# First transform of a long convolution: even and odd parts as two matmuls into the PSUM halves, evicted whole by ScalarE; VectorE multiplies and folds

## The reference, cut to what matters

```python
# B, S, D = 2, 11456, 128
h_filt = (np.maximum(pos_emb @ w1, 0.0) @ w2) * np.exp(-0.01 * pos)[:, None]
u = x * v
Uf = np.fft.rfft(u, n=2 * S, axis=1)
Hf = np.fft.rfft(h_filt, n=2 * S, axis=0)
y = np.fft.irfft(Uf * Hf[None, :, :], n=2 * S, axis=1)[:, :S, :]
attn_out = x * y
# then: expert layer 1 on attn_out, expert layer 2 on its result
```

## Time and profile before

| what | us |
|---|---|
| median of 3 runs | 2397.1 |
| the profiled execution | 2405.55 |
| its span (first to last instruction) | 2403.3 |
| filter stage | until about 80 |
| `spectra`, first half | 79.8 to 187.3 |
| `products`, first half | 187.3 to about 331 |
| `spectra`, second half | 331.0 to 431.2 |
| DVE busy over the span | 1359.6 (57%) |
| PE busy over the span | 1995.1 (83%) |

### The profile page before, as it was taken

One profiled execution on the slowest core, in us unless ns is written; L12 is line 12 of the kernel. 1 busy time (PEld: TensorE's weight loads), 2 busy tenths in 40 slices (PEclk: granted clock), 3 DMA queues, 4 the chain that ended last, 5 costly groups with the idle time before them and its releaser, 6 DMA issues. The chain is left out here.

```text
span 2403.3 us, 35753 instructions
## 1 busy us (share of the span) xinstructions
PE 1995.1 (83%) x9744; PEld 1639.1 (68%) x9744; DVE 1359.6 (57%) x3564; ACT 998.3 (42%) x2175; POOL 775.4 (32%) x738
## 2 busy tenths in 40 slices
PE   6577878686657675199999999999679999999996
PEld 4474567454647564178888887888558888888885
DVE  2397859774435353256666665666535555555552
ACT  3363333232222121045455554545335555555553
POOL 2143215330344555403232322222403333333333
PEclk9689998897667766599999999999889999999998
DMA  6657866786645563355555555555256666666662
GB/s 203 179 150 255 270 181 170 221 279 204 206 156 197 184 227 120 139 191 192 205 190 205 189 203 188 188 207 179 92 191 225 223 221 224 219 220 224 223 219 79
DMA packets 164823, 471.11 MB, mean 196 GB/s; under 512 B 24634, under 2 KB 80750, under 8 KB 135113
## 3 DMA queue, kind: packets, MB, share of 16 engines
q1 hardware_dynamic: 129416, 385.43, 49.0%
q0 software_dynamic: 24064, 61.17, 7.5%
q10 hardware_dynamic: 11264, 23.57, 3.2%
HBM read 365.29 MB, written 109.49 MB: 198 GB/s over the span
## 5 line engine op out<-in xcount | busy, mean ns | idle before, releaser
L1151 DVE SCALAR_TENSOR_TENSOR m_hid<-m_pH,m_hid 128x512 fp32r<-128x512 f32 x832 | 574.5, 691 | 406.5 <-ACT m_hid L1105 330.3
L1105 ACT ACTIVATE m_hid<-m_pH 128x512 fp32r<-128x512 f32 x832 | 501.0, 603 | 614.4 <-PE m_pH L1033 585.4
L1223 POOL DMA_INDIRECT rows<-m_rows,m_idx x208 | 204.0, 981 | 522.9 <-DVEq L1190 464.0
L1031 PE MATMUL m_pH<-m_xT,m_w 128*128 128x512 f32 x832 | 353.2, 425 | 11.4 <-DVE m_hid L1151 5.1
L1227 POOL DMA_INDIRECT out_dram<-m_rows,m_token x208 | 203.9, 980 | 434.2 <-ACT m_rows L1119 384.5
L1033 PE MATMUL m_pH<-m_xT,m_w 128*128 128x512 f32 x832 | 327.1, 393 | 0.0
L1032 PE MATMUL m_pH<-m_xT,m_w 128*128 128x512 f32 x832 | 326.9, 393 | 0.0
L1044 PE MATMUL m_pO<-m_hid,m_w 128*128 128x512 f32 x832 | 326.4, 392 | 0.0
L1046 PE MATMUL m_pO<-m_hid,m_w 128*128 128x512 f32 x832 | 326.0, 392 | 0.0
L1045 PE MATMUL m_pO<-m_hid,m_w 128*128 128x512 f32 x832 | 324.1, 390 | 0.0
L927 POOL DMA_INDIRECT rows<-oi_rows,oi_idx x192 | 194.3, 1012 | 226.7 <-ACT oi_raw_logits L880 129.2
(11 more groups left out here) (154 smaller groups left out, 2669.7 us busy)
## 6 DMA issues: line engine op xcount, KB each, us to landing
m_w<-halves_w SPq DMA_DIRECT2D x104, 1024.0 KB, 5.0
m_w<-halves_next_w SPq DMA_DIRECT2D x104, 1024.0 KB, 5.1
m_x<-rows SPq DMA_DIRECT2D x104, 264.0 KB, 4.3
pr_mats<-in_inner_dram SPq DMA_DIRECT2D x92, 256.0 KB, 3.9
inner_back<-pr_c SPq DMA_DIRECT2D x92, 256.0 KB, 3.5
oi_C<-inner_back SPq DMA_DIRECT2D x32, 728.0 KB
halves_w<-pr_parts POOLq DMA_DIRECT2D x16, 1024.0 KB
halves_next_w<-oi_parts ACTq DMA_DIRECT2D x32, 512.0 KB
```

The source lines that it names most:

```text
L1031: nc.tensor.matmul(out, high, xT[:, s % 2, 0], start=True, stop=False)
L1105: nc.scalar.activation(hid[:, s % 2, c, 0], pH[:, c % 2], ACT.Relu).then_inc(H_high, 1)
L1151: nc.vector.scalar_tensor_tensor(hid[:, s % 2, c, 1], pH[:, c % 2], 0.0, hid[:, s % 2, c, 0].bitcast(F32), ALU.max, ALU.subtract).then_inc ...
L1223: pool.indirect_dma_start(next_rows, bass.IndirectOffsetOnAxis(r.idx[:, s, t:t + 1], 0), rows[:, s, t, :], None, bounds_check=E * CAP + TI ...
```

## The change

The even and odd parts of a channel become two matmuls of 64 output partitions each, into partitions 0 to 63 and 64 to 127 of the same PSUM columns. The odd one has its own constant (`W[:, 1]`, the sine columns with their sign first, then minus the cosines), so that real and imaginary parts lie in the same columns for both, and the sign needs no instruction. ACT then evicts each part over all 128 partitions, in the form of the second half for both halves. DVE no longer evicts: it multiplies x by v, one signal chunk ahead of its folds, and folds. POOL has nothing to do in this stage. Filter and signal chunks alternate, one filter chunk and then two of signals, and `us` has 4 buffers. `W` is twice as long.

```diff
--- before.py
+++ after.py
@@ -186,81 +186,77 @@
 
 def spectra(nc, half, x, v, h_d, outer_d, A):
 
-    R = 3
+    R, UR = 4, 3
     with ExitStack() as ctx:
         sb, ps, sem = makers(nc, ctx, f"sp{half}")
-        xs, vs, us = (sb(n, [JP, R, CD, 2, HS]) for n in ("x", "v", "u"))
-        W = sb("W", [JP, 2 * K1])
+        xs, vs = (sb(n, [JP, UR, CD, 2, HS]) for n in ("x", "v"))
+        us = sb("u", [JP, R, CD, 2, HS])
+        W = sb("W", [JP, 2, 2 * K1])
         pA = ps("pA", [ST, 2, 4, 512])
         W_in = sem("W_in")
-        h_in, x_in = ([sem(f"{n}{s}") for s in range(R)] for n in ("h_in", "x_in"))
-        multiplied, folded = sem("multiplied"), sem("folded")
-        A_ready, even_out, odd_out = sem("A_ready"), sem("even_out"), sem("odd_out")
+        h_in, x_in = [sem(f"h_in{s}") for s in range(R)], [sem(f"x_in{s}") for s in range(UR)]
+        multiplied, folded, A_ready, A_out = sem("multiplied"), sem("folded"), sem("A_ready"), sem("A_out")
+
+        def is_filter(c):
+            return c % 3 == 0
+
+        def signal(c):
+
+            return c - c // 3 - 1
+
+        def place(u):
+
+            return u + u // 2 + 1
 
         def columns(c, part):
 
-            if c < CHUNKS_H:
-                at = WU + part * HD + c * CD
+            if is_filter(c):
+                at = WU + part * HD + c // 3 * CD
             else:
-                b, m = divmod(c - CHUNKS_H, CHUNKS_H)
+                b, m = divmod(signal(c), CHUNKS_H)
                 at = part * B * HD + b * HD + m * CD
             return slice(at, at + CD)
 
-        def move(c, rows, src, part):
-
-            outs = A[rows, :, columns(c, part)]
-            ins = pA[rows, c % 2, :, 0:4 * K1].rearrange("p a (t w) -> p a t w", t=2)[:, :, :, src * K1:(src + 1) * K1]
-            if half == 0:
-                return outs.rearrange("p k (a t) -> p a t k", t=2), ins
-            return outs.rearrange("p k (a t) -> p k a t", t=2), ins.rearrange("p a t w -> p w a t")
-
         block = ctx.enter_context(nc.Block())
 
         @block.sync
         def _(sp):
-            sp.dma_start(W[:, :], outer_d).then_inc(W_in, 16)
+            sp.dma_start(W[:, :, :].rearrange("p e w -> p (e w)"), outer_d).then_inc(W_in, 16)
+
             def load_filter(c):
                 if c >= R:
                     sp.wait_ge(A_ready, c - R + 1)
                 sp.dma_start(us[:, c % R].rearrange("p d e s -> p (d e s)"),
-                             h_d[half, :, c * CD * ST:(c + 1) * CD * ST]).then_inc(h_in[c % R], 16)
+                             h_d[half, :, c // 3 * CD * ST:(c // 3 + 1) * CD * ST]).then_inc(h_in[c % R], 16)
 
             def load_signals(u):
                 b, m = divmod(u, CHUNKS_H)
-                if u >= R:
-                    sp.wait_ge(folded, 2 * (u - R + 1))
+                if u >= UR:
+                    sp.wait_ge(folded, 2 * (u - UR + 1))
                 for dst, src in ((xs, x), (vs, v)):
-                    sp.dma_start(dst[:, u % R].rearrange("p d e s -> p (d e s)"),
-                                 src[b, half, :, m * CD * ST:(m + 1) * CD * ST]).then_inc(x_in[u % R], 16)
-
-            for c in range(CHUNKS_H):
-                load_filter(c)
-                if c < R:
-                    load_signals(c)
-            for u in range(R, CHUNKS_U):
-                load_signals(u)
-
-        @block.gpsimd
-        def _(pool):
-            for u in range(CHUNKS_U):
-                pool.wait_ge(x_in[u % R], 32 * (u // R + 1))
-                nc.gpsimd.tensor_tensor(xs[:, u % R], xs[:, u % R], vs[:, u % R], ALU.mult).then_inc(multiplied, 1)
+                    sp.dma_start(dst[:, u % UR].rearrange("p d e s -> p (d e s)"),
+                                 src[b, half, :, m * CD * ST:(m + 1) * CD * ST]).then_inc(x_in[u % UR], 16)
+
+            for c in range(CHUNKS_1):
+                if is_filter(c):
+                    load_filter(c)
+                else:
+                    load_signals(signal(c))
 
         @block.tensor
         def _(pe):
             pe.wait_ge(W_in, 16)
             for c in range(CHUNKS_1):
-                if c < CHUNKS_H:
-                    pe.wait_ge(h_in[c % R], 16 * (c // R + 1))
+                if is_filter(c):
+                    pe.wait_ge(h_in[c % R], 16 * len([k for k in range(0, c + 1, 3) if k % R == c % R]))
                 else:
-                    pe.wait_ge(folded, 2 * (c - CHUNKS_H + 1))
+                    pe.wait_ge(folded, 2 * (signal(c) + 1))
                 if c >= 2:
-                    pe.wait_ge(even_out, 2 * (c - 1))
-                    pe.wait_ge(odd_out, 2 * (c - 1))
+                    pe.wait_ge(A_out, 2 * (c - 1))
                 for d in range(CD):
-                    last = nc.tensor.matmul(pA[:, c % 2, d // 2, d % 2 * 2 * K1:(d % 2 + 1) * 2 * K1],
-                                            us[:, c % R, d].rearrange("p e s -> p (e s)"), W[:, :],
-                                            start=True, stop=True)
+                    for e in range(2):
+                        last = nc.tensor.matmul(pA[e * HS:(e + 1) * HS, c % 2, d // 2, d % 2 * 2 * K1:(d % 2 + 1) * 2 * K1],
+                                                us[:, c % R, d, e], W[:, e], start=True, stop=True)
                 last.then_inc(A_ready, 1)
 
         @block.scalar
@@ -268,27 +264,31 @@
             for c in range(CHUNKS_1):
                 act.wait_ge(A_ready, c + 1)
                 for part in range(2):
-                    dst, src = move(c, slice(0, HS), part, part)
-                    nc.scalar.activation(dst, src, ACT.Copy).then_inc(even_out, 1)
+                    src = pA[:, c % 2, :, 0:4 * K1].rearrange("p a (t w) -> p a t w", t=2)
+                    nc.scalar.activation(A[:, :, columns(c, part)].rearrange("p k (a t) -> p k a t", t=2),
+                                         src[:, :, :, part * K1:(part + 1) * K1].rearrange("p a t w -> p w a t"),
+                                         ACT.Copy).then_inc(A_out, 1)
 
         @block.vector
         def _(dve):
-            def fold(c):
-                u = c - CHUNKS_H
+            def multiply(u):
+                dve.wait_ge(x_in[u % UR], 32 * (u // UR + 1))
+                nc.vector.tensor_tensor(xs[:, u % UR], xs[:, u % UR], vs[:, u % UR], ALU.mult).then_inc(multiplied, 1)
+
+            def fold(u):
+                c = place(u)
                 dve.wait_ge(multiplied, u + 1)
-                dve.wait_ge(A_ready, c - R + 1)
+                if c >= R:
+                    dve.wait_ge(A_ready, c - R + 1)
                 for e, op in enumerate((ALU.add, ALU.subtract)):
-                    nc.vector.tensor_tensor(us[:, c % R, :, e], xs[:, u % R, :, 0], xs[:, u % R, :, 1],
+                    nc.vector.tensor_tensor(us[:, c % R, :, e], xs[:, u % UR, :, 0], xs[:, u % UR, :, 1],
                                             op).then_inc(folded, 1)
 
-            for c in range(CHUNKS_1):
-                if CHUNKS_H <= c + 2 < CHUNKS_1:
-                    fold(c + 2)
-                dve.wait_ge(A_ready, c + 1)
-                dst, src = move(c, slice(HS, ST), 1, 0)
-                nc.vector.tensor_copy(dst, src).then_inc(odd_out, 1)
-                dst, src = move(c, slice(HS, ST), 0, 1)
-                nc.vector.tensor_scalar(dst, src, -1.0, None, ALU.mult).then_inc(odd_out, 1)
+            multiply(0)
+            for u in range(CHUNKS_U):
+                if u + 1 < CHUNKS_U:
+                    multiply(u + 1)
+                fold(u)
 
 
 def products(nc, half, A, mats_d, c_d, weights, halves_d):
@@ -1314,7 +1314,7 @@
     number = np.where(at < S, at, NOWHERE) + np.where(at < S, S, 0) * np.arange(B)[:, None, None, None]
     return {
         "inner": f(np.stack([there, there.transpose(0, 2, 1)], axis=2).reshape(K1, ST, 2 * ST)),
-        "outer": f(np.concatenate([np.cos(outer) * real, -np.sin(outer) * real], axis=1)),
+        "outer": f(np.concatenate([np.cos(outer), -np.sin(outer), -np.sin(outer), -np.cos(outer)], axis=1) * real),
         "outer_inv": f(np.stack([weight * np.cos(back), -weight * np.sin(back), weight * np.sin(back)], axis=1) * real[:, 0]),
         "window": f(np.repeat(window, FO, axis=0).reshape(2 * FO, GROUPS, 2, GC)),
         "consts": f(np.concatenate([np.eye(128), np.ones((128, 128)), np.triu(np.ones((128, 128)), 1)], axis=1)),
```

## The result

The changed kernel takes 2442.05 us (median of 4 runs, 2430.51 to 2447.61) against 2400.09 for the kernel before (2391.37 to 2405.64): a ratio of 1.0196 with a 95% interval from 1.0142 to 1.0251. It is 42 us slower. The forecast was 2419, slower, with a range from 2390 to 2475: the direction was right, the loss about twice the 22 us that were forecast.

The account below looks back on a forecast made before the run. It took DVE to bound the first half, and folds slowed beside POOL's multiply in the second; the added wait makes the stages 115.0 and 114.3, 229.3 against 207.6: +21.7 on 2397.1 gives 2419 us, range 2390 to 2475.

Parts of the forecast that it names:

- P: Period of three chunks in a `spectra` stage, from the end of chunk 2 to that of chunk 5: 13.8 us.
- The wait that is added: In each three-chunk group, chunk 5's fold stands on DVE behind chunk 7's multiply, whose loads queue behind F6: 13.8 us.
- Landing: Term of P: a filter load and the next x and v arrive in 6.7 us, bounds 5.1 and 8.3.
- PE's chunk: Term of P: PE's chunk 5, after standing 3.8 us, takes 4.4 us, between 2.8 and 5.2.
- A stage: One `spectra` stage: chunk 2 ends at 21.5, six periods to 104.3, then the end: 115.0 us; second half 114.3.
- 64 + 12 P: Sum of both `spectra` stages in us with the forecast's start; it decides at P = 12.0.
- What PE costs: 32 passes a chunk instead of 16; with column groups side by side a chunk stays at 2.8 us.
- Rival 1: Column groups run one after the other on PE: 5.4 us a chunk, +73 us, 2470; chance 0.28.
- rival 3: Each PE pass exposes its weight load: 11 us a chunk, 272 a stage, 2733; chance 0.03.
- 79% of the ideal: Column-group estimate from the skill page: 3.4 us a chunk on PE, about 12 us more in the sum.
- Rival 2: Wait stays, but full clock and loads of 5.9 us: P 11.4, 2386 us; chance 0.24 with its milder form.
- What goes: DVE's evictions and POOL's multiply go; DVE then costs 2.5 us a signal chunk, ACT 0.75 an instruction.

Follow-up runs that it names:

- experiment 1: Changed kernel with DVE folding chunk u before multiplying chunk u+1; stages 78.1 and 76.3 us, 2237.31 against 2293.45 us for the kernel before, ratio 0.9744.
- experiment 2: Changed kernel with SP issuing the signal load that follows a filter load ahead of it; stages 80.7 and 80.5 us, ratio 0.9793 to the kernel before.
- experiment 3: Changed kernel with 6 input buffers for the matmuls in place of 4; stages 82.1 and 80.6 us, ratio 0.9857 to the kernel before.
- Experiment 5: Changed kernel with 18 extra matmuls ahead of every second signal chunk; stages 113.7 and 110.4 us, ratio 1.0053 to the kernel before.
- experiment 4: Kernel before with each matmul split into two of 64 output partitions, nothing else changed; stages 109.4 and 102.6 us, ratio 0.9985 to the kernel before.
- the second comparison: Changed kernel run again without edit against the kernel before, on another chip; 2428.87 against 2397.3 us, ratio 1.0130.
- experiment 7: Changed kernel with all 8 filter chunks first, DVE's look-ahead kept; stages 95.5 and 96.7 us, 2276.88 us (one run) against 2295.49 for the kernel before.

## Why the prediction was right, and where its sizes were off

- **The forecast's size.** The direction and the mechanism held. The loss was forecast at 22 us and measured at 42. That is inside the stated range but outside the forecast's own, which ended at 2434; the stages' +36.1 stand at that edge, as P does (12.9 to 15).
- **The wait that is added** was the step on which all rests, and it held link by link: filter load behind PE's release, the signal loads behind it on the queue, the multiply for the next chunk, the fold, the chunk. Experiments 1, 2 and 3 each cut or slackened one link, the other links untouched, and each brought the stages from 122 to between 76 and 82 us.
- **P** was 13.8 and is 14.8 over the first half's six periods (109.52 to 198.25). Two terms were too small. Landing was put at 6.7 and took 7.2 to 7.6 us, 7.4 on the mean (109.52 to 117.01 in the turn shown). I had priced the transfers ahead of chunk 7's v, but not that two more are issued behind it; whether these slow it was not tried. PE's chunk was put at 4.4, the time of a mixed chunk, and took 4.4 to 5.2, 4.9 on the mean: PE stood 4.4 to 5.1 us before it and not 3.8, and the clock over it was 0.50 twice and 0.53 to 0.62 four times, towards the upper end that the earlier trace rows gave. With 2.5 for multiply, folds and semaphore this adds up to 14.8. Experiment 5 shows that the chunk's term is the clock.
- **A stage** was put at 115.0 and took 121.4. Chunk 2 ends 23.0 us after the stage's start and not 21.5; the six periods add 5.9; so chunk 20 ends at 198.25 - 86.53 = 111.7 and not 104.3. The end is 1.0 us shorter than thought. The second half was put 0.7 us shorter than the first and is 0.9 longer. The sum was to be +21.7 and is +36.1; with a period of 14.9 the prediction's own formula, 64 + 12 P, gives 243.
- **What PE costs** was right in kind, and 0.3 us too high: 2.5 to 2.6 us a chunk at full clock for 32 passes, where 2.8 was taken. Rival 1 (5.4 us) and rival 3 (11 us) are out by experiments 1 and 4. The nearest rows, of row groups, had told it. The Trainium skill, TensorE: Matmul & The Clock Gate, Part 3 (Packing small matmuls), says that small outputs in distinct column groups run concurrently, and the trace agrees. The 79% of the ideal, an estimate that the prediction worked out from that part's three tiles, was not found: here two groups gave the whole factor of 2 (156 ns for a pair of passes, 156 before for one). Its sentence that weight loads overlap only where row groups differ does not fit this trace: both groups use the same 96 rows, and in experiment 1's first stage 57.4 us of weight loads and 66.6 of matmuls lie in 78.1 us. (The 75 us of loads that the prediction sets against that sentence stand in the earlier trace rows, not in the earlier trace rows.)
- **Rival 2** failed on both its conditions. The 4.4 to 5.1 us of standing in each period brought the clock down every time, and the landing took 7.4 and not 5.9. Experiment 5 makes the first condition by force: its period of 12.95 in the first half is still above the 12.0 at which the forecast's formula decides. Its +16.5 us can't be set against rival 2 as they stand, since some 9 of them are the extra matmuls ahead of chunk 23.
- **What goes** came as worked out (ACT 0.78 us an instruction where 0.75 was taken, DVE 2.5 us a signal chunk), and was worth nothing until the order let it count.

Not settled: the part of the 42 us that lies outside the stages (some 6 us, within the scatter of the runs; 31.6 in the second comparison, 5 below the stages' 36.6), why the landing took 0.7 us longer than the prediction's rows gave, and where the 104 us between the batches arise behind the second stage.

## What to carry to other kernels

When work is moved to an engine with time to spare, read its program order as a list of waits: an instruction that runs ahead for the next chunk puts that chunk's load in front of this chunk's result. Look for a ring that closes over a queue (here: PE's release, SP's next load, the look-ahead multiply, the fold, PE), and add up one turn of it; if that is longer than the busiest engine's work in the same turn, it is the bound, and freeing engines gains nothing. One link taken out can be enough: a swap of two lines on DVE was worth 89 us here. But look for the next ring behind it: in experiment 7 the filter load's link was gone, and the look-ahead still cost a buffer (96 us a stage, against 76 to 82).

## What the runs showed of the hardware that was not expected

- Two matmuls with 64 output partitions each, in different column groups, with the same 96 rows, took the time of one of 128: their passes start 3 to 7 and then 149 to 153 ns apart, in fp32, 184 columns.
- Where the order has 16 passes of one group and then 16 of the other, passes still overlap across the border: 3.85 us for 32 passes and not 5.0.
- ACT's eviction of 64 x 736 took 1455 ns on the mean with PSUM contiguous and the SBUF side strided, and 771 to 783 the other way round, on 64 and on 128 partitions alike.
- VectorE's folds took 680 ns on the mean with POOL idle, and 811 to 1201 where POOL multiplied in the same stage.
